# Attention's product with the values, in two runs for each pair of heads instead of one key chunk a slot

## The chip, the core and the metric

One core of one Trainium2 chip (trn2). The time is microseconds of device time for one execution. The core's engines are TensorE (PE in the profile; its weight loads are PEld), VectorE (DVE), ScalarE (ACT), GpSimd (POOL) and SyncE (SP), which issues the DMAs. Each works through its own list of instructions in order; semaphores join them. Matmuls write to PSUM, which has eight banks.

## What is computed

Attention over 4 batches and 8 heads with 576 positions and a head size of 64, followed by two feed-forward layers over the 2304 tokens of width 512. The attention part, cut to what matters here:

```python
scores = scale * np.matmul(q, k.transpose(0, 1, 3, 2)) + bias      # bias: 8 x 576 x 576, one for each head
scores = scores - np.max(scores, axis=-1, keepdims=True)
attn = np.exp(scores)
attn = attn / (np.sum(attn, axis=-1, keepdims=True) + 1e-09)
return np.matmul(attn, v)
```

The first layer is `g = h * cos(h)` between two products, the second an RMS norm with a gated product. Everything is float32.

## The kernel before

The kernel runs in stages: the bias (to about 66 us), attention (about 67 to 366 us), the first layer, the second layer. The change is in the attention stage alone, `attention_phase`.

Attention goes through 16 pairs of heads. The two heads of a pair have 5 query tiles each (four of 128 rows and one of 64), so a pair is 10 tiles and 10 **slots**. In slot s of pair n the engines do this, each in the order written:

- PE: `score` computes tile s into one of two PSUM bank pairs (`scores[s % 2]`), in four matmuls of 288 columns (L505). It first waits until VectorE has finished tile s-2 (semaphore `biased`). Then `turn` transposes the normalised probabilities of the tile of four slots ago (`T_LAG`), with four transposes (L531) and for tiles 5 to 9 a fifth (L527). It waits until the tile is normalised, and until ScalarE has copied the tile two before it out of PSUM (semaphore `copied`), since `turned` has two banks. Then `mix` multiplies one chunk of 128 keys with the values for one half (288) of the queries.
- VectorE: `guard` and `invert` of tile s-2 (L654, L659), `normalise` of tile s-3 where it is an even one (L411; GpSimd has the odd ones), and `add_bias` of tile s (L647), which waits for `scored`.
- ScalarE: `exps` of tile s (L597), which waits for `add_bias` of tile s, then `keep` of tile s-4 (L611, tile 9 also L609), the copy of the transposed tile out of PSUM.
- GpSimd: `normalise` of the odd tiles, and the high and low parts of q and k of what comes next (L346, L350, L356).

Five chunks make one half: chunks 0 to 3 go as two matmuls, one for each head, each of which writes 64 of the 128 PSUM partitions (L550, shape 128*64 in the profile; each shows as two records), and the fifth, with the 64 keys left of both heads, as one matmul over all 128 (L554, shape 128*128). The two halves are 10 chunks for 10 slots: half 0 of pair n-1 in slots 3 to 7, half 1 in slots 8, 9 and 0 to 2 of the next pair. VectorE copies a finished half to `X` (`keep_mixed`, L668) in slots 8 and 3, and the transposed end keys (`keep_end`, L664) after the `add_bias` of slot 4.

After the last pair PE goes through ten slots without scores, then does the first product of the next layer (`chunks.first_h`, L821 to L823), then the last three chunks of half 1. VectorE has `keep_mixed` of the second last pair, `keep_end`, the split of the next layer's input (`features.high`, `features.low`, L808 and L815) and then the last two `keep_mixed`.

Of the kernel before, what the change touches and what calls it, by code (L numbers as in the profile page):

```python
# [29 lines left out]
NQ = 5  # L30
TILES = 2 * NQ
HS = S // 2
QPAD = NQ * P
EXP_LAG, T_LAG = 2, 4
EARLY_TILES = 3


# [21 lines left out]
def after_waits(eng, passed):  # L59


    eng.sem_inc(passed, 1)


def rows_of(qt):

    return P if qt < NQ - 1 else S - (NQ - 1) * P


def bias_phase(nc, sb, sem_of, ins, bias_scratch, att):  # L70
# [43 lines left out]

    EARLY = -(-EARLY_TILES * P // (KINDS * ROWS))
    assert N % 2 == 0 and EARLY % 2 == 0
# [10 lines left out]
    with nc.Block() as block:  # L127

        @block.sync
        def _(sp):  # L130
# [27 lines left out]
            for stored in (*bias_stored[0], *bias_stored[1]):  # L158
                sp.wait_ge(stored, 8 * EARLY)
            for s in range(EARLY_TILES):  # L160
                att.load_bias(sp, 0, s, True, 0)
# [206 lines left out]
def attention_phase(nc, sb, sem_of, att, features, weights, chunks, bank_pairs, banks):  # L368
    ctx = ExitStack()
    X, ident, values, bias = att.X, att.ident, att.values, att.bias  # L370
    scored, biased, mixed_ready = att.scored, att.biased, att.mixed_ready
# [9 lines left out]
    probs_t_end = [sb(ctx, f"probs_t_end{i}", [P, S], F32) for i in range(2)]  # L381
# [8 lines left out]
    copied = sem_of("a_copied")  # L390
    end_copied = sem_of("a_end_copied")
    last_end_copied = sem_of("a_last_end_copied")
    mixed_copied = sem_of("a_mixed_copied")
# [3 lines left out]
    LAST = PAIRS - 1  # L397
# [3 lines left out]
    def normed_of(n, s):  # L401

        return (pool_normed if s in POOL_TILES else dve_normed), n * (TILES // 2) + (s // 2 + 1)
# [10 lines left out]
    with nc.Block() as block:  # L414

        @block.sync
        def _(sp):
            for stored in (*att.bias_stored[0], *att.bias_stored[1]):
                sp.wait_ge(stored, 8 * (GROUPS // KINDS))
            for s in range(EARLY_TILES, TILES):  # L420
                att.load_bias(sp, 0, s, True, 0)
# [73 lines left out]
        @block.tensor  # L495
        def _(pe):
            def score(n, s, first):
                h, qt = s // NQ, s % NQ
                if qt == 0:
                    pe.wait_ge(att.prepared[h], n + 1)  # L500
                if not (first and s < 2):
                    pe.wait_ge(biased, n * TILES + (s - 1))
                for half in range(2):
                    for part, k_part in ((0, att.k_high[h]), (1, att.k_low[h])):
                        last = nc.tensor.matmul(scores[s % 2][:, half, 0:HS], att.q_parts[h][:, qt * P:(qt + 1) * P],  # L505
                                                k_part[:, half * HS:(half + 1) * HS], start=(part == 0), stop=(part == 1))
                last.then_inc(scored, 1)

            def turn(n, s, first):

                h, qt = s // NQ, s % NQ
                rows = rows_of(qt)
                pe.wait_ge(*normed_of(n, s))
                if not (first and s < 2):
                    pe.wait_ge(copied, n * TILES + (s - 1))
                if s == NQ and not first:
                    pe.wait_ge(end_copied, n)
                if h == 1:

                    both = by_heads[qt][0:rows, :, :, :].rearrange("p h a b -> p (h a b)")[:, S - D:S + D]  # L520
                    end = turned[s % 2] if qt == NQ - 1 else turned_end
                    at = (NQ - 1) * rows if qt == NQ - 1 else qt * P
                    pe.wait_ge(*normed_of(n, qt))
                if qt == NQ - 1 and not first:
                    after_waits(pe, pe_passed)
                if h == 1:
                    nc.tensor.transpose(end[:, at:at + rows], both, ident[0:rows, 0:rows])  # L527
                flat = probs[s].rearrange("p a b -> p (a b)")
                for c in range(NQ - 1):
                    at = h * D + c * P  # L530
                    last = nc.tensor.transpose(turned[s % 2][:, c * rows:(c + 1) * rows], flat[0:rows, at:at + P],  # L531
                                               ident[0:rows, 0:rows])
                last.then_inc(turned_ready, 1)

            def mix(n, parity, half, c, first):

                if c == 0:
                    if half == 0:
                        pe.wait_ge(att.values_in[parity], n * 8 + (16 - 8 * parity))

                        pe.wait_ge(copied, n * TILES + (NQ + 3))
                    else:
                        pe.wait_ge(copied, (n + 1) * TILES)
                        pe.wait_ge(last_end_copied, n + 1)
                    if not (first and half == 0):
                        pe.wait_ge(mixed_copied, n * 2 + half)
                queries = slice(half * HS, (half + 1) * HS)
                if c < NQ - 1:
                    for h in range(2):
                        nc.tensor.matmul(mixed[h * D:(h + 1) * D, 0:HS], values[parity][:, c, h, :],  # L550
                                         probs_t[parity][:, h, c, queries], start=(c == 0), stop=False)
                else:
                    pe.wait_ge(end_copied, n + 1)
                    nc.tensor.matmul(mixed[:, 0:HS], values[parity][:, c, :, :].rearrange("p h d -> p (h d)"),  # L554
                                     probs_t_end[parity][:, queries], start=False, stop=True).then_inc(mixed_ready, 1)

            def slot(n, parity, s, step, compute=True):

                if compute:
                    score(n, s, step == 0)  # L560
                if s < T_LAG:
                    if step > 0:
                        turn(n - 1, TILES - T_LAG + s, False)
                elif compute:
                    turn(n, s - T_LAG, step == 0)
                if s < 3:
                    if step > 1:
                        mix(n - 2, parity, 1, s + 2, False)
                elif step > 0:
                    half, c = divmod(s - 3, NQ)  # L570
                    mix(n - 1, 1 - parity, half, c, step == 1)

            def pair(n, parity, step):
                for s in range(TILES):
                    slot(n, parity, s, step)

            pe.wait_ge(att.ident_ready, 2)
            pe.wait_ge(att.pad_ready, 2)
            pair(0, 0, 0)
            pair(1, 1, 1)  # L580
            with pe.Fori(1, PAIRS // 2) as m:
                pair(m * 2, 0, 2)
                pair(m * 2 + 1, 1, 2)
            for s in range(TILES):
                slot(PAIRS, 0, s, 2, compute=False)

            pe.wait_ge(biased, PAIRS * TILES)
            chunks.first_h(pe)
            for c in range(2, NQ):
                mix(LAST, 1, 1, c, False)  # L590

        @block.scalar
        def _(act):
# [44 lines left out]
        def _(dve):  # L638
# [22 lines left out]
            def keep_end(n, parity):  # L661

                dve.wait_ge(turned_ready, n * TILES + (TILES - 1))
                dve.tensor_copy(probs_t_end[parity][:, 0:(NQ - 1) * P], turned_end[:, :]).then_inc(end_copied, 1)  # L664

            def keep_mixed(n, half):
                dve.wait_ge(mixed_ready, n * 2 + (half + 1))
                dve.tensor_copy(X[:, bass.ds(n * S + half * HS, HS)], mixed[:, 0:HS]).then_inc(mixed_copied, 1)  # L668

            def back(n, parity, s, by):  # L670

                return (n, parity, s - by) if s >= by else (n - 1, 1 - parity, TILES + s - by)

            def pair(n, parity, step, hp=None):

                for s in range(TILES):
                    m, _, r = back(n, parity, s, EXP_LAG)
                    m3, _, r3 = back(n, parity, s, EXP_LAG + 1)

                    if step > 1 and s == 3:  # L680
                        keep_mixed(n - 2, 1)
                    if step > 0 and s == 8:
                        keep_mixed(n - 1, 0)
                    if s >= EXP_LAG or step > 0:
                        guard(m, r)
                    if (s >= EXP_LAG + 1 or step > 0) and r3 not in POOL_TILES:
                        normalise(dve, m3, r3, dve_normed)
                    if s >= EXP_LAG or step > 0:
                        invert(m, r)
                    if hp is not None:  # L690
                        dve.wait_ge(att.bias_in[s], (hp + 1) * 16)
                    add_bias(n, s, step == 0)
                    if step > 0 and s == 4:
                        keep_end(n - 1, 1 - parity)

            pair(0, 0, 0, hp=0)
            pair(1, 1, 1)
# [788 lines left out]
```

## Time and profile before

| | |
|---|---|
| median of 3 runs | 1233.66 us (1233.5 to 1233.79) |
| the profiled execution | 1233.59 us |
| its span in the trace | 1231.8 us |
| PE busy | 1192.9 us (97%) |
| PEld busy | 1076.7 us (87%) |
| DVE busy | 701.6 us (57%) |
| ACT busy | 500.5 us (41%) |
| POOL busy | 483.1 us (39%) |

The span is the time from the first to the last instruction in the trace; some 1.8 us lie around it. The busy shares are means over stages of different kinds, so the attention stage has to be read by itself. An engine's busy time is the time in which at least one of its instructions was under way; the ends of matmuls are modelled.

### The profile page before, as it was taken

The numbers are of one execution on the slowest core, as the hardware profiler recorded it, in microseconds if no ns is written. First come the engines' busy times: TensorE is split into PE (matmuls) and PEld (weight loads), VectorE is DVE, ScalarE is ACT, GpSimd is POOL, SyncE is SP. The second block draws the span as 40 slices with busy tenths as digits, with TensorE's granted clock in tenths as the row PEclk, the third lists the DMA queues.
The fourth block names the chain that finished last, engine by engine and source line by source line (L and its number), as shares of the span: only waits on it lengthen the run. The fifth ranks groups of instructions, "written<-read, shape, count | busy, mean of one in ns | idle before, by whom it ended". The sixth has DMA issues, their size and how long they took to land. (4 is left out here: it accounts for less than half of the span.)

```text
span 1231.8 us, 21813 instructions
## 1 busy us (share of the span) xinstructions
PE 1192.9 (97%) x7464; PEld 1076.7 (87%) x7464; DVE 701.6 (57%) x1540; ACT 500.5 (41%) x1034; POOL 483.1 (39%) x515
## 2 busy tenths in 40 slices
PE   5789999999989999999999999999999999999998
PEld 2367777777759999999999999999999999999998
DVE  8977777777759977868686788554002020110201
ACT  6967777777733333334333333211111111111111
POOL 3056666666665452433325254572111111111111
PEclk9989999999989999999999999999999999999999
DMA  5854425252124300000000001241000000000000
GB/s 176 248 167 123 157 79 184 71 166 94 61 67 120 86 2 1 0 0 0 0 0 0 0 17 52 69 137 35 1 1 26 0 26 0 0 26 0 26 0 26
DMA packets 46534, 69.06 MB, mean 56 GB/s; under 512 B 3712, under 2 KB 27424, under 8 KB 46496
## 3 DMA queue, kind: packets, MB, share of 16 engines
q1 hardware_dynamic: 46496, 68.60, 17.9%
q8 instruction: 19, 0.31, 0.1%
q14 instruction: 19, 0.16, 0.0%
HBM read 53.25 MB, written 15.34 MB: 56 GB/s over the span
## 5 line engine op out<-in xcount | busy, mean ns | idle before, releaser
L823 PE MATMUL banks<-x_high,w_low_rest 128*128 128x384 f32 x672 | 224.8, 334 | 0.0
L822 PE MATMUL banks<-x_low,w_high_rest 128*128 128x384 f32 x672 | 224.6, 334 | 0.0
L821 PE MATMUL banks<-x_high,w_high_rest 128*128 128x384 f32 x672 | 224.6, 334 | 0.0
L1370 DVE TENSOR_TENSOR X<-X,banks 128x384 f32<-128x384 f32 x72 | 39.8, 552 | 299.1 <-PE banks L823 299.1
L1389 POOL TENSOR_TENSOR product_low<-X,product_high 128x384 fp32r<-128x384 f32 x72 | 72.8, 1011 | 346.0 <-ACT product_high L1332 346.0
L1187 POOL TENSOR_TENSOR product_low<-g,product_high 128x384 fp32r<-128x384 f32 x96 | 102.4, 1066 | 236.7 <-ACT product_high L1069 236.7
L821 PE MATMUL bank<-product_high,w_high_rest 128*128 128x384 f32 x480 | 162.2, 338 | 0.8 <-POOL product_low L1187 0.8
L823 PE MATMUL bank<-product_high,w_low_rest 128*128 128x384 f32 x480 | 160.7, 335 | 0.0
L822 PE MATMUL bank<-product_low,w_high_rest 128*128 128x384 f32 x480 | 160.6, 335 | 0.0
L647 DVE CUSTOM_DVE_ANT_0 probs<-banks,bias 128x576 f32<-128x576 f32 (+1 forms) x160 | 119.8, 749 | 61.1 <-PE banks L505 59.1
L597 ACT ACTIVATE probs<-probs,neg_max 128x576 f32<-128x576 f32 (+1 forms) x160 | 124.4, 777 | 71.8 <-DVE neg_max L647 71.1
L1097 ACT ACTIVATE angle<-angle,quarter 128x384 f32<-128x384 f32 x96 | 59.3, 617 | 202.6 <-DVE angle L1129 202.6
L823 PEld LDWEIGHTS banks<-x_high,w_low_rest 128*128 128x128 f32 x672 | 126.2, 188 | 0.0
L822 PEld LDWEIGHTS banks<-x_low,w_high_rest 128*128 128x128 f32 x672 | 126.2, 188 | 0.0
L821 PEld LDWEIGHTS banks<-x_high,w_high_rest 128*128 128x128 f32 x672 | 126.2, 188 | 0.0
L505 PE MATMUL banks<-k_high,q_parts 128*128 128x288 f32 x320 | 111.0, 362 | 2.5 <-PEq L127 2.5
L411 POOL TENSOR_SCALAR probs<-probs,inv_total 128x576 f32<-128x576 f32 (+1 forms) x80 | 59.5, 744 | 131.4 <-DVE inv_total L659 130.8
L505 PEld LDWEIGHTS banks<-k_high,q_parts 128*128 128x128 f32 x320 | 61.5, 192 | 56.5 <-DVE neg_max L647 37.5
L1319 ACT ACTIVATE X<-banks 128x384 f32<-128x384 f32 x71 | 34.9, 492 | 185.4 <-PE banks L823 185.4
L1332 ACT ACTIVATE product_high<-X 128x384 fp32r<-128x384 f32 x72 | 37.8, 525 | 172.5 <-DVE X L1370 172.5
L1124 DVE SCALAR_TENSOR_TENSOR angle<-turns,angle 128x384 f32<-128x384 int32 x96 | 105.5, 1099 | 3.1
L550 PE MATMUL bank<-probs_t,values 128*64 128x288 f32 x512 | 90.3, 435 | 4.7 <-DVE X L668 4.7
(113 smaller groups left out, 2547.4 us busy)
## 6 DMA issues: line engine op xcount, KB each, us to landing
raw_qk<-in_qk SPq DMA_DIRECT2D x32, 576.0 KB, 3.7
bias_scratch<-bias_stage SPq DMA_DIRECT2D x36, 288.0 KB, 3.1
bias<-bias_scratch SPq DMA_DIRECT2D x32, 288.0 KB, 3.1
w_raw<-in_w_out SPq DMA_DIRECT2D x28, 256.0 KB, 2.6
values<-in_v SPq DMA_DIRECT2D x16, 320.0 KB, 4.0
w_raw<-in_w_in SPq DMA_DIRECT2D x16, 256.0 KB, 3.0
out_t<-X SPq DMA_DIRECT2D x5, 768.0 KB, 3.5
w_raw<-in_w_gate SPq DMA_DIRECT2D x12, 256.0 KB, 3.0
```

What stands on the lines that cost most here:

```text
L411: eng.tensor_scalar(probs[s][0:rows], probs[s][0:rows], inv_total[0:rows, s:s + 1], scalar2, ALU.mult, op1).then_inc(normed, 1)
L505: last = nc.tensor.matmul(scores[s % 2][:, half, 0:HS], att.q_parts[h][:, qt * P:(qt + 1) * P], k_part[:, half * HS:(half + 1) * HS], star ...
L550: nc.tensor.matmul(mixed[h * D:(h + 1) * D, 0:HS], values[parity][:, c, h, :], probs_t[parity][:, h, c, queries], start=(c == 0), stop=False)
L597: act.activation(probs[s][0:rows], probs[s][0:rows], ACT.Exp, bias=neg_max[0:rows, s:s + 1], scale=-1.0, accum_out=total[0:rows, s:s + 1]) ...
L647: dve.tensor_tensor_reduce(out=probs[s][0:rows], in0=scores[s % 2][0:rows, :, 0:HS], in1=bias[s][0:rows, :, :], scale=-float(D) ** -0.5, s ...
L821: nc.tensor.matmul(out, high, x_high, start=start, stop=False)
L822: nc.tensor.matmul(out, high, x_low, start=False, stop=False)
L823: return nc.tensor.matmul(out, low, x_high, start=False, stop=stop)
L1097: act.activation(angle[:, :], angle[:, :], ACT.Sin, bias=quarter[:, :]).then_inc(cos_ready, 1)
L1124: dve.scalar_tensor_tensor(angle[:, :], turns[:, :], -TWO_PI_LOW, angle[:, :], ALU.mult, ALU.add).then_inc(fine_angle, 1)
L1187: pool.tensor_tensor(gl[f % 2][:, :], g[:, :], gh[f % 2][:, :].bitcast(F32), ALU.subtract).then_inc(g_split, 1)
L1389: pool.tensor_tensor(sl[f % 2][:, :], s, sh[f % 2][:, :].bitcast(F32), ALU.subtract).then_inc(s_split, 1)
```

## The change

`mix` now issues all five chunks of a half in one go. Half 0 of pair n-1 runs in slot 4 of pair n and half 1 in slot 9, each after the slot's `score` and `turn`. The other eight slots have no product with the values. VectorE's `keep_mixed` moves from slots 3 and 8 to slots 1 and 6, and `keep_end` from behind the `add_bias` of slot 4 to the head of slot 3. After the last pair PE has five slots without scores instead of ten, then `first_h`, then the whole of the last half.

```diff
+MIX_SLOTS = (4, 9)
@@ tensor engine
-            def mix(n, parity, half, c, first):
-
-                if c == 0:
-                    if half == 0:
-                        pe.wait_ge(att.values_in[parity], n * 8 + (16 - 8 * parity))
-
-                        pe.wait_ge(copied, n * TILES + (NQ + 3))
-                    else:
-                        pe.wait_ge(copied, (n + 1) * TILES)
-                        pe.wait_ge(last_end_copied, n + 1)
-                    if not (first and half == 0):
-                        pe.wait_ge(mixed_copied, n * 2 + half)
+            def mix(n, parity, half, first):
+
+                pe.wait_ge(att.values_in[parity], n * 8 + (16 - 8 * parity))
+                pe.wait_ge(copied, n * TILES + (NQ + 3) if half == 0 else (n + 1) * TILES)
+                if not (first and half == 0):
+                    pe.wait_ge(mixed_copied, n * 2 + half)
                 queries = slice(half * HS, (half + 1) * HS)
-                if c < NQ - 1:
+                for c in range(NQ - 1):
                     for h in range(2):
                         nc.tensor.matmul(mixed[h * D:(h + 1) * D, 0:HS], values[parity][:, c, h, :],
                                          probs_t[parity][:, h, c, queries], start=(c == 0), stop=False)
-                else:
-                    pe.wait_ge(end_copied, n + 1)
-                    nc.tensor.matmul(mixed[:, 0:HS], values[parity][:, c, :, :].rearrange("p h d -> p (h d)"),
-                                     probs_t_end[parity][:, queries], start=False, stop=True).then_inc(mixed_ready, 1)
+                pe.wait_ge(end_copied, n + 1)
+                if half == 1:
+                    pe.wait_ge(last_end_copied, n + 1)
+                nc.tensor.matmul(mixed[:, 0:HS], values[parity][:, NQ - 1, :, :].rearrange("p h d -> p (h d)"),
+                                 probs_t_end[parity][:, queries], start=False, stop=True).then_inc(mixed_ready, 1)
@@ slot
-                if s < 3:
-                    if step > 1:
-                        mix(n - 2, parity, 1, s + 2, False)
-                elif step > 0:
-                    half, c = divmod(s - 3, NQ)
-                    mix(n - 1, 1 - parity, half, c, step == 1)
+                if step > 0 and s in MIX_SLOTS:
+                    mix(n - 1, 1 - parity, MIX_SLOTS.index(s), step == 1)
@@
-            for s in range(TILES):
+            for s in range(MIX_SLOTS[0] + 1):
                 slot(PAIRS, 0, s, 2, compute=False)
 
             pe.wait_ge(biased, PAIRS * TILES)
             chunks.first_h(pe)
-            for c in range(2, NQ):
-                mix(LAST, 1, 1, c, False)
+            mix(LAST, 1, 1, False)
@@ vector engine
-                    if step > 1 and s == 3:
+                    if step > 1 and s == 1:
                         keep_mixed(n - 2, 1)
-                    if step > 0 and s == 8:
+                    if step > 0 and s == 6:
                         keep_mixed(n - 1, 0)
+                    if step > 0 and s == T_LAG - 1:
+                        keep_end(n - 1, 1 - parity)
...
                     add_bias(n, s, step == 0)
-                    if step > 0 and s == 4:
-                        keep_end(n - 1, 1 - parity)
```

## Rows read from the trace of the kernel before

**Rows 1.** Stretches: busy us and instructions of each engine, PE clock, DMA share, GB/s

```profile
74.00:86.00 12.00, 10.00 (x74) 8.49 (x72) 11.73 (x40) 10.88 (x27) 9.73 (x11) 1.00 0.36 122
193.00:210.70 17.70, 17.70 (x123) 12.53 (x121) 13.46 (x50) 13.13 (x32) 11.95 (x13) 1.00 0.65 204
357.00:364.00 7.00, 6.50 (x22) 4.75 (x24) 0.35 (x1) 0.00 (x0) 1.72 (x2) 0.51 0.29 77
```

**Rows 2.** PE timeline, first score matmul of slot 0, two pairs: start us, us, what

```profile
97.69 0.40 PE L505 MATMUL banks<-k_high,q_parts 128*128 128x288 f32 x1
115.38 0.40 PE L505 MATMUL banks<-k_high,q_parts 128*128 128x288 f32 x1
```

**Rows 3.** PE timeline: a slot with a two-head chunk, one with the end chunk

```profile
211.59 0.29 PE L505 MATMUL banks<-k_low,q_parts 128*128 128x288 f32 x1
211.72 0.60 PE L531 MATMUL bank<-ident,probs 128*128 128x128 f32 x4
212.25 0.71 PE L550 MATMUL bank<-probs_t,values 128*64 128x288 f32 x4
212.89 0.40 PE L505 MATMUL banks<-k_high,q_parts 128*128 128x288 f32 x1
...
217.57 0.65 PE L554 MATMUL bank<-probs_t_end,values 128*128 128x288 f32 x2
...
218.19 0.29 PE L505 MATMUL banks<-k_low,q_parts 128*128 128x288 f32 x1
```

**Rows 4.** PE timeline behind the last pair: four two-head chunks back to back

```profile
350.09 2.16 PE L550 MATMUL bank<-probs_t,values 128*64 128x288 f32 x16 [0.18 <-DVE X L668]
...
352.18 0.75 PE L554 MATMUL bank<-probs_t_end,values 128*128 128x288 f32 x2
```

**Rows 5.** Timeline of pairs 0 and 1, slots without any product with the values

```profile
74.62 0.78 ACT L597 ACTIVATE probs<-probs,neg_max 64x576 f32<-64x576 f32 x1 [0.18 <-DVE neg_max L647]
...
75.40 0.57 ACT L611 ACTIVATE probs_t<-bank 128x512 f32<-128x512 f32 x1
...
76.12 0.63 PE L531 MATMUL bank<-ident,probs 128*128 128x128 f32 x4 [0.44 <-ACT probs_t L611]
...
84.47 0.78 ACT L597 ACTIVATE probs<-probs,neg_max 128x576 f32<-128x576 f32 x1
...
85.73 0.76 ACT L597 ACTIVATE probs<-probs,neg_max 128x576 f32<-128x576 f32 x1
```

**Rows 6.** Timeline of VectorE and the exp behind it, steady pairs and pair 15

```profile
212.10 0.75 DVE L647 CUSTOM_DVE_ANT_0 probs<-banks,bias 64x576 f32<-64x576 f32 x1 [0.45 <-PE banks L505]
...
212.79 0.07 DVE L647 DVE_READ_ACCUMULATOR2_ANT neg_max<- 64x1 f32 x1
...
212.90 0.78 ACT L597 ACTIVATE probs<-probs,neg_max 64x576 f32<-64x576 f32 x1 [0.22 <-DVE neg_max L647]
...
213.39 0.14 DVE L654 TENSOR_SCALAR guarded<-total 128x1 f32<-128x1 f32 x1
...
213.95 0.73 DVE L647 CUSTOM_DVE_ANT_0 probs<-banks,bias 128x576 f32<-128x576 f32 x1
...
342.29 0.46 DVE L668 COPY X<-bank 128x288 f32 x1
...
343.12 0.76 DVE L647 CUSTOM_DVE_ANT_0 probs<-banks,bias 128x576 f32<-128x576 f32 x1
```

**Rows 7.** Timeline of the end of the stage

```profile
345.53 0.33 PE L527 MATMUL bank<-ident,probs 128*128 128x128 f32 x1
...
349.86 0.68 DVE L664 COPY probs_t_end<-bank 128x512 f32<-128x512 f32 x1
...
357.50 0.75 PE L550 MATMUL bank<-probs_t,values 128*64 128x288 f32 x2 [4.56 <-DVE X L668]
...
366.42 0.19 PEld L821 LDWEIGHTS banks<-x_high,w_high_head 128*128 128x128 f32 x1 [1.25 <-issue]
```

**Rows 8.** VectorE's normalise in the view of line L411: duration ns min/median/max

```profile
L411 DVE TENSOR_SCALAR probs<-probs,inv_total x80: 501/510/1233, 72.3 to 346.4; 128x576 f32<-128x576 f32 x64, 64x576 f32<-64x576 f32 x16
```

## The prediction

> **What bounds the kernel now.** The page gives PE 97% of the span, but the change touches one stage only, so I read the stretches by stage first, then the timeline of single slots, then the few places where the trace already shows what the changed kernel will do everywhere. In a steady pair PE is busy for all of its 17.70 us, while DVE has 13.46, ACT 13.13 and POOL 11.95 [rows 1]. Pair follows pair every 17.69 us (97.69 to 115.38) [rows 2]. So today PE sets the pace and waits for nobody; every slot is about 1.8 us long, and each of the others idles a little in each slot. Note for later that PE's weight loads cover only 12.53 of 17.70.
>
> Where does PE's time go? In a slot with a two-head chunk the transposes start at 211.72, the chunk at 212.25 (0.53 later) and the next scores at 212.89 (0.64 later) [rows 3]. In a run of four such chunks, which the tail of the stage has, they take 350.09 to 352.18, 2.09 us, or 0.52 each [rows 4]. Each single chunk pays at its two borders as well: the end chunk, which has the shape of its neighbours, goes from its start at 217.57 to the second score matmul at 218.19, 0.62 for two records and one score matmul of 0.13 (211.59 to 211.72), so 0.49 of streaming [rows 3].
>
> **The change part by part.**
>
> *PE's own work.* A slot with a two-head chunk is 0.36 longer than one with the end chunk counted at its streaming time: 0.10 ahead of it (0.53 where four transposes at 0.11 need 0.43), 0.15 in it (0.64 less 0.49) and 0.11 in the slower first score behind it [rows 3]. Eight such slots a pair pay 2.9 us. In the new form a run pays once: 0.10 ahead, 2.09 for the four chunks instead of 1.96, and 0.10 in the end chunk (its two records take 0.75 behind a run and 0.65 else [rows 3, 4]), some 0.4 a half and 0.8 a pair. PE's own work falls by 2.1 us, to 15.6 a pair. This part is sure; the same instructions ran in the same order in the tail.
>
> *What the others must do in the meantime.* Now the slots differ: eight have 0.96 to 1.07 us of PE work, two have about 3.7. DVE and ACT cannot store work for the long slots: `scores` has two buffers, so when PE goes into a run they have at most the tile just scored and the one before it. And in the short slots they are slower than PE. Pair 0 and the first slots of pair 1 show exactly such slots, without any product: in 74 to 86 us DVE is busy 11.73 of 12, ACT 10.88, PE 10.00 [rows 1]. There PE waits for ACT's copy: the exp of a slot starts at 74.62, the copy behind it at 75.40, and the turn of two slots later can start at 76.12 [rows 5]. So **exp of slot s to turn of slot s+2 is 1.50**, and a backlogged ACT starts an exp every 1.26 (84.47 to 85.73) [rows 5].
>
> From these I walk once round the loop. Half A, from the turn of slot 4 to the turn of slot 9:
> - turn of slot 4 to the run: 0.53. The run: 2.09. End chunk to the last score matmul of slot 5: 0.62 + 2 x 0.13 + 0.10 behind a run = 0.98. Last score matmul to `add_bias` on an idle DVE: 0.51 (211.59 to 212.10). Sum 4.11 [rows 3, 4, 6].
> - `add_bias` to exp of slot 5: 0.80 (212.10 to 212.90) [rows 6].
> - slot 5 to slot 6, with `keep_mixed` now at the head of slot 6: 0.69 to the end of `add_bias` (212.10 to 212.79) and 0.83 from the copy to the next `add_bias` (342.29 to 343.12), 1.52, and the exp follows at the same distance [rows 6].
> - slot 6 to 7: ACT's 1.26. Exp of slot 7 to turn of slot 9: 1.50 [rows 5].
> - Half A: 4.11 + 0.80 + 1.52 + 1.26 + 1.50 = 9.19.
>
> Half B, from the turn of slot 9 to that of the next slot 4: a fifth transpose (0.11) makes the first term 4.22; then 0.80; slot 0 to 1 has both `keep_mixed` and an even tile to normalise, 0.69 + 0.46 + 0.56 (guard at 213.39 to `add_bias` at 213.95) = 1.71 [rows 6]; then 1.26 and 1.50. Half B: 9.49.
>
> **One pair: 18.68 us, 0.99 longer than now** (17.69), although PE has 2.1 less to do. PE would be idle for 3.1 of it. I take 18.65.
>
> *Other waits.* `keep_end` stands in DVE's slot 3 now, 0.68 ahead of that slot's `add_bias`; that `add_bias` is not on the loop (slot 2's exp is), and PE needs the copy only 2.09 into the run. The run of half 1 needs the last copy of slot 3, five slots before. `keep_mixed` never waits, because a run is through before the next slot's scores. POOL has 11.95 in 18.65; its normalise of tile 5, needed by the turn of slot 9, comes after slot 7's `invert`, and a POOL instruction takes 0.92 in the mean (11.95 for 13 [rows 1]), against 2.3 us until that turn (0.80 and 1.50). The loads of q, k, values and bias wait for the same steps as now, with a longer pair. All these at nothing; if one more POOL step lands ahead of it, the price is another 0.92 at most, in a pair where that happens.
>
> *The page on packing.* ACT's copies get PSUM free at a rate of 10 x 1.26 = 12.6 us a pair, below PE's new 15.6 [rows 5]. The Trainium skill, TensorEngine Tiling (Array Packing), PSUM Bottleneck, says that tiling quickens TensorE but not the evacuation, which may become the limit. Taken as a rate it would not bind here and the pair would be 15.6; what I expect is its delay, not its rate.
>
> *Start.* In pair 1 the exp of slot 2 starts at 85.73 in both kernels, so the turn of slot 4 comes at 87.23 [rows 5]. Fourteen pairs on it is 87.23 + 14 x 18.65 = 348.33; the turn of slot 9 of the last pair 9.19 later, 357.52; behind its run (0.64 + 2.09 + 0.59) the turn of tile 6, 360.84. Now that turn is at 345.53 [rows 7]. **15.3 us lost by then.**
>
> *Tail.* Now the stage needs 20.9 us from that turn to the next stage's first load at 366.42. Within it VectorE starts `keep_end` 4.33 in (349.86), finishes the split of the input at about 357.0 (`keep_mixed`'s 0.46 [rows 6] ahead of PE's start at 357.50), 11.5 in, and PE waits 4.56 for that `keep_mixed`, because half 1's first chunks stand ahead of `first_h`; then it works at half the clock, 0.51 granted [rows 1, 7]. In the new order no chunk stands there. Slots without chunks let `keep_end` start about 2.3 in (estimate: two turns, with 1.5 from turn over copy to turn, by the durations of [rows 5]), the split ends 7.1 later, as now (349.86 to 357.0), at 9.4; `first_h` follows it piece by piece and ends at 10.1; the run 2.1, end chunk, `keep_mixed` and the exit together 1.7: about 13.9. **7.0 us won.** If the clock falls to 1.2 GHz as it does now (half of 2.4), `first_h`'s end and the run take twice as long and the gain is 4.2. I take 7.0, because PE no longer stands still for 4.56 but does a quarter of `first_h` for each of the four parts that VectorE has split (L815), and the clock kept 1.00 with 2 of 12 us idle in pair 0 [rows 1].
>
> Sum against the profiled execution: 1233.59 + 15.3 - 7.0 = 1241.9. The median of the runs is 0.07 above that execution, so 1242.0.
>
> **The rivals.**
>
> *PE stays the bound (faster).* If DVE and ACT keep up, because PE's waits in pair 0 are few (0.44 is the one in [rows 5]) and the loop is shorter than I add up, a pair takes 15.6. Then fourteen pairs save 14 x 2.1 = 29.4, pair 1 about 1, the tail 7: 1196. For it: PE is the one engine without idle time. Against: the loop's terms are all measured, and would have to be 3 us a pair too long. It decides where half a loop falls under 7.8. The Trainium skill, Perfetto Trace Analysis, Identifying the Most-Contended Engine, gives this result: improve the engine of highest occupancy first, though it wants TensorE judged by its weight loads, whose share here is 12.53 of 17.70 [rows 1].
>
> *The bubbles are smaller.* If the loop is 0.5 to 1 us shorter, because in places a `keep_mixed` or the exp of slot 6 is hidden behind the wait for the scores, the pair is as long as now and the tail's gain is left over: 1227 to 1235.
>
> *The loop is longer.* VectorE's normalise takes 0.51 by the median, but up to 1.23 [rows 8], which I put down to GpSimd working beside it, and in the new order the normalise of slots 1 and 7 is on the loop. By my order POOL is idle or waiting at both, but if one of them is hit, each pair gains 0.6 more, 14 x 0.6 = 8: 1250. The half clock in the tail alone gives 1245.
>
> **How the numbers follow.** Loop as walked: 0.70, own range 1236 to 1248 (0.35 a pair either way and the clock). PE the bound or nearly: 0.09. Smaller bubbles: 0.11. Longer loop: 0.10. 0.2% is 2.5 us, about what a measurement of this kernel can tell from no change. Faster by more than that: 0.09 and half of the smaller bubbles, 0.14. Within it: 0.07. Slower: 0.79. The range takes in the main case and most of both neighbours: 1231 to 1251.
>
> **What would show it.** Right: a steady pair of about 18.65 us with PE busy some 15.6; PE idle ahead of the turns of slots 4 and 9, released by ACT's copy (L611), in all some 3 us a pair; DVE idle for about 1.5 to 2.5 us ahead of the `add_bias` of slots 5 and 0, released by the scores; runs of 2.09 for L550; the turn of tile 6 behind the last pair near 360.8 and the next stage 13 to 17 us after it. Wrong: a pair below 17.7, or idle time that stands elsewhere (POOL's normalise, DMA), or L550 records longer than 0.26 apart in a run.

## The result and the profile after

The changed kernel takes 1239.71 us, median of 4 runs (1239.44 to 1240.08); the kernel before, on the same chip, 1233.58. The ratio is 1.0056, with a 95% interval of 1.0044 to 1.0068: slower by 0.56%, or some 6.9 us by the ratio (6.1 by the two medians). The profiled execution took 1239.96 us, its span 1238.2, so 6.4 us more than the span before.

The head of the page of the changed kernel, busy time of each engine:

```profile
span 1238.2 us, 21829 instructions
PE 1176.5 (95%) x7464; PEld 1079.6 (87%) x7464; DVE 698.5 (56%) x1540; ACT 494.1 (40%) x1034; POOL 482.6 (39%) x515
```

The same number of instructions on each of these engines, 16.4 us less of PE, and a longer time: PE did save work and now stands still elsewhere. The same view as [rows 1], one steady pair (18.52 us) and the tail:

```profile
193.00:211.52 18.52, 16.84 (x123) 12.88 (x122) 13.23 (x48) 12.75 (x31) 11.93 (x14) 1.00 0.66 197
363.00:370.00 7.00, 5.91 (x34) 3.26 (x32) 5.72 (x6) 2.09 (x4) 6.75 (x7) 1.00 0.41 112
```

PE was busy for all of 17.70 us and now is for 16.84 of 18.52. Who waits for whom in the pairs between 140 and 317 us (total in us, times, longest):

```profile
POOL probs L412 <- DVE inv_total L650: 60.4, 48, 2.7
ACT probs L588 <- DVE neg_max L638: 53.5, 48, 2.4
DVE probs L638 <- PE banks L506: 43.8, 19, 2.7
...
PE bank L532 <- ACT probs_t L602: 5.9, 10, 0.6
PE bank L528 <- ACT probs_t L602: 3.9, 10, 0.5
```

The third row shows it best. VectorE waits for scores only 19 times, twice a pair, but for 2.3 us each: once behind every run. Before, it waited a little in many slots, 0.45 in the one shown in [rows 6]. The last two rows are new, PE waiting for ScalarE's copies; before, that was to be seen only in pairs 0 and 1 [rows 5].

Now one half of the loop, from the turn of slot 4 (198.82) to the turn of slot 9 (207.96), in the timeline of the changed kernel. L532 and L528 are the transposes, L545 the two-head chunks, L550 the end chunk, L638 `add_bias`, L588 exp:

```profile
198.82 0.63 PE L532 MATMUL bank<-ident,probs 128*128 128x128 f32 x4
...
199.38 2.16 PE L545 MATMUL bank<-probs_t,values 128*64 128x288 f32 x16
...
201.47 0.75 PE L550 MATMUL bank<-probs_t_end,values 128*128 128x288 f32 x2
...
202.97 0.76 DVE L638 CUSTOM_DVE_ANT_0 probs<-banks,bias 128x576 f32<-128x576 f32 x1 [1.99 <-PE banks L506]
...
203.77 0.78 ACT L588 ACTIVATE probs<-probs,neg_max 128x576 f32<-128x576 f32 x1 [2.23 <-DVE neg_max L638]
...
204.38 0.29 PE L506 MATMUL banks<-k_low,q_parts 128*128 128x288 f32 x1
...
204.47 0.76 DVE L638 CUSTOM_DVE_ANT_0 probs<-banks,bias 128x576 f32<-128x576 f32 x1
...
205.27 0.63 PE L532 MATMUL bank<-ident,probs 128*128 128x128 f32 x4 [0.60 <-ACT probs_t L602]
205.27 0.78 ACT L588 ACTIVATE probs<-probs,neg_max 128x576 f32<-128x576 f32 x1
...
206.52 0.76 ACT L588 ACTIVATE probs<-probs,neg_max 128x576 f32<-128x576 f32 x1
...
207.96 0.30 PE L528 MATMUL bank<-ident,probs 128*128 128x128 f32 x1
```

Read it downwards: turn to run 0.56, the run 2.09, end chunk to `add_bias` 1.50, to the exp 0.80, to the next exp 1.50 (the copy of a finished half stands between the two `add_bias`), to the next 1.25, and from there to the turn 1.44. Sum 9.14. While VectorE (1.99) and ScalarE (2.23) wait, PE is in its run; then PE waits for them.

The tail, which answers to [rows 7]:

```profile
359.57 0.27 PE L528 MATMUL bank<-ident,probs 128*128 128x128 f32 x1
...
361.79 0.69 DVE L655 COPY probs_t_end<-bank 128x512 f32<-128x512 f32 x1 [1.56 <-PE bank L532]
...
363.40 4.95 DVE L806 TENSOR_TENSOR x_low<-X,x_high 128x384 fp32r<-128x384 f32 x4
...
365.18 0.41 PE L812 MATMUL banks<-x_high,w_high_head 128*128 128x384 f32 x1 [0.20 <-DVE x_low L806]
...
369.12 2.16 PE L545 MATMUL bank<-probs_t,values 128*64 128x288 f32 x16
...
372.78 0.41 PE L812 MATMUL banks<-x_high,w_high_head 128*128 128x384 f32 x1 [0.82 <-PEq L415]
```

The turn of tile 6 behind the last pair is at 359.57, 14.0 us later than before (345.53). From there the next stage starts after 13.2 us instead of 20.9. 14.0 - 7.7 = 6.3, and the spans differ by 6.4.

### The profile page after: what moved, and what is told of

Same layout as the page of the kernel before. It is cut to its first block and busy times, and to the rows that moved or that the text cites. A ratio compares the mean times of both kernels' runs of the same rounds, so it can differ in the third digit from the quotient of the medians.

```text
span 1238.2 us, 21829 instructions
## 1 busy us (share of the span) xinstructions
PE 1176.5 (95%) x7464; PEld 1079.6 (87%) x7464; DVE 698.5 (56%) x1540; ACT 494.1 (40%) x1034; POOL 482.6 (39%) x515
## 5 line engine op out<-in xcount | busy, mean ns | idle before, releaser
L638 DVE CUSTOM_DVE_ANT_0 probs<-banks,bias 128x576 f32<-128x576 f32 (+1 forms) x160 | 119.4, 747 | 78.0 <-PE banks L506 71.3
L588 ACT ACTIVATE probs<-probs,neg_max 128x576 f32<-128x576 f32 (+1 forms) x160 | 123.6, 773 | 90.7 <-DVE neg_max L638 88.4
L506 PE MATMUL banks<-k_high,q_parts 128*128 128x288 f32 x320 | 107.9, 352 | 3.0 <-PEq L128 2.5
L532 PE MATMUL bank<-ident,probs 128*128 128x128 f32 (+1 forms) x640 | 91.1, 264 | 14.9 <-ACT probs_t L602 9.5
L812 PEld LDWEIGHTS bank<-product_high,w_high_rest 128*128 128x128 f32 x480 | 90.1, 188 | 2.1 <-POOL product_low L1178 1.1
```

Source lines behind the costliest of these rows:

```text
L588: act.activation(probs[s][0:rows], probs[s][0:rows], ACT.Exp, bias=neg_max[0:rows, s:s + 1], scale=-1.0, accum_out=total[0:rows, s:s + 1]) ...
L638: dve.tensor_tensor_reduce(out=probs[s][0:rows], in0=scores[s % 2][0:rows, :, 0:HS], in1=bias[s][0:rows, :, :], scale=-float(D) ** -0.5, s ...
L812: nc.tensor.matmul(out, high, x_high, start=start, stop=False)
```

## The experiments

The length of a pair is taken in each trace as the distance of the `add_bias` of slot 5 in successive pairs, mean over pairs 3 to 15. Times are medians; each ratio is to the kernel before, run on the same chip (1232.39 us beside the first four experiments, 1232.93 beside the last four), with its 95% interval.

| kernel | time, us | ratio | pair, us |
|---|---|---|---|
| before | 1233.58 | 1 | 17.70 |
| changed | 1239.71 | 1.0056 (1.0044 to 1.0068) | 18.53 |
| before, new tail | 1228.01 | 0.9964 (0.995 to 0.9979) | 17.70 |
| changed, `keep_mixed` in slots 3 and 8 | 1231.06 | 0.9989 (0.9979 to 0.9998) | 17.94 |
| changed, copy ahead of exp | 1222.80 | 0.9927 (0.9911 to 0.9944) | 17.25 |
| before, copy ahead of exp | 1232.78 | 1.0002 (0.9993 to 1.0012) | 17.70 |
| four runs a pair | 1224.43 | 0.9934 (0.9918 to 0.9951) | 17.48 |
| four runs, copy ahead of exp | 1209.62 | 0.9811 (0.9795 to 0.9827) | 16.47 |
| changed, runs of half the length | 1212.72 | 0.9835 (0.9819 to 0.9852) | 16.60 |
| changed, copy ahead of exp, `keep_end` behind slot 3 | 1220.55 | 0.9897 (0.9881 to 0.9914) | 17.09 |

The theory was that a loop of waits sets the pair, and that the tail is a gain of its own. The rival was that some engine's amount of work does.

**The tail alone.**

```diff
--- before
-            for s in range(TILES):
+            for s in range(8):
                 slot(PAIRS, 0, s, 2, compute=False)
             pe.wait_ge(biased, PAIRS * TILES)
             chunks.first_h(pe)
-            for c in range(2, NQ):
+            for c in range(NQ):
                 mix(LAST, 1, 1, c, False)
```

> The kernel before, with the new tail alone: one key chunk a slot in all pairs, and behind the last pair the slots end with half 0, then comes first_h, then the whole of half 1. Theory (the tail is a gain of its own, which hides part of what the runs cost): PE no longer waits 4.56 us for keep_mixed ahead of first_h, first_h follows the split of the input, the last half runs at full clock; the stage ends about 5 us earlier (366.4 to about 361.6), so about 1229. Rival (the tail's gain needs the runs, or the split of the input on VectorE alone sets the stage's end): no more than 1 us, 1232.5 to 1233.7.

Measured: 1228.01, 4.4 us less. Its timeline has the last half at 357.82 and GpSimd, which starts the next stage with the others (366.41 in the kernel before), at 361.44:

```profile
357.82 2.16 PE L550 MATMUL bank<-probs_t,values 128*64 128x288 f32 x16
...
359.91 0.75 PE L554 MATMUL bank<-probs_t_end,values 128*128 128x288 f32 x2
...
361.44 0.10 POOL L1206 MEMSET quarter<- 128x1 f32 x1 [2.57 <-POOLq L414]
```

The last half ran in 2.09 (357.82 to 359.91), as the run behind the last pair in [rows 4] did, and the granted clock from 357 to 361.4 is 1.00. So this gain of the tail does not need the runs; it hid part of their price in the result. It is 5.0 us on the timeline (366.41 to 361.44), of the 7.7 that the changed kernel wins there. The other 2.7 I put down to the slots that have no chunk: there `keep_end` starts 2.2 us behind the turn of tile 6 instead of 4.3.

**`keep_mixed` off the loop.**

```diff
--- changed kernel
-                    if step > 1 and s == 1:
+                    if step > 1 and s == 3:
                         keep_mixed(n - 2, 1)
-                    if step > 0 and s == 6:
+                    if step > 0 and s == 8:
                         keep_mixed(n - 1, 0)
```

> The changed kernel with keep_mixed back in VectorE's slots 3 and 8 instead of 1 and 6; the runs stay. Theory (a loop of waits from the turn of one run's slot over add_bias, exp and copy to the turn of the next run's slot sets the pair): keep_mixed stands on that loop in slots 1 and 6. Without it slot 5 to 6 costs ScalarE's 1.26 instead of 1.52 and slot 0 to 1 costs 1.26 instead of 1.71, so the pair falls by 0.7, from 18.52 to about 17.8, and the time by 14 to 15 times that, to about 1229. Rival (PE's or VectorE's amount of work sets the pair): the same copies are made, no change, 1239 to 1240.

Measured: 1231.06, and 17.94 a pair, 0.59 less than the changed kernel. The same copies, made two slots later, are worth 8 us (the ratios differ by 0.0067). An engine's amount of work cannot explain that; their place on the loop can. The walk had 0.7 and 1229.

**ScalarE's copy ahead of its exp**, in the changed kernel and in the one before.

```diff
--- changed kernel, and kernel before
                 for s in range(TILES):
-                    exps(n, s)
                     if s >= T_LAG:
                         keep(n, parity, s - T_LAG)
                     elif not first:
                         keep(n - 1, 1 - parity, TILES - T_LAG + s)
+                    exps(n, s)
```

> The changed kernel, with ScalarE's two steps of each slot in the other order: the copy of tile s-4 out of PSUM first, then the exp of tile s. Nothing is added or left out. Theory (the loop of waits): the copy that frees the bank for the turn two slots later no longer stands behind the exp of the tile just scored. By the same walk half A falls to about 8.3 and half B to about 8.2, the pair from 18.5 to about 16.5, the time to about 1210 (1206 to 1218). Rival (ScalarE's or VectorE's amount of work, or the wait for the scores, sets the pair): ScalarE has the same work, no change within 2 us of 1239.7.

> The kernel before with the same swap of ScalarE's copy and exp. Theory: with one chunk a slot PE is the bound and waits for nobody, so the order on ScalarE is worth nothing in the steady pairs; only pair 0 and the first slots of pair 1, where PE waits for the copies, get up to 3 us shorter: 1230.5 to 1233.8. Rival (the order on ScalarE is worth something by itself): 1225 or less, or slower because each exp now starts later.

Measured: 1222.80 and 17.25 a pair in the changed kernel, so 1.28 us a pair for an order alone; 1232.78 and the same 17.70 in the kernel before. The swap is worth nothing where PE is the bound and 16 us where the loop is (1.0056 less 0.9927). But the walk had promised 2.0 a pair, and 1222.80 is outside its range of 1206 to 1218. The trace of the swapped kernel shows what came up in its place, at the turn of slot 4:

```profile
189.92 0.69 DVE L655 COPY probs_t_end<-bank 128x512 f32<-128x512 f32 x1
...
190.52 0.14 DVE L645 TENSOR_SCALAR guarded<-total 128x1 f32<-128x1 f32 x1
190.58 0.51 DVE L412 TENSOR_SCALAR probs<-probs,inv_total 128x576 f32<-128x576 f32 x1
...
191.15 0.66 PE L532 MATMUL bank<-ident,probs 128*128 128x128 f32 x4 [0.25 <-DVE probs L412]
```

The turn waits for VectorE's normalise, and that stands behind `keep_end`, which the change had moved to the head of slot 3. So I moved it behind the slot's `add_bias`:

```diff
--- changed kernel with the copy ahead of the exp
-                    if step > 0 and s == T_LAG - 1:
-                        keep_end(n - 1, 1 - parity)
...
                     add_bias(n, s, step == 0)
+                    if step > 0 and s == T_LAG - 1:
+                        keep_end(n - 1, 1 - parity)
```

> The changed kernel with ScalarE's copy ahead of the exp (1222.8, 17.23 a pair instead of the 16.5 of my walk), and keep_end moved behind the add_bias of slot 3. In the trace of that kernel the turn of slot 4 waits for VectorE's normalise of tile 0, which stands behind keep_end (0.69) in slot 3. Theory (with the copy off the loop, VectorE's slot 3 is what the turn of slot 4 waits for): the wait of 0.25 to 0.3 goes and the pair falls to about 16.95, the time to about 1218.5. Rival (the scores that wait for VectorE's add_bias set that turn anyway): no change, 1222 to 1223.5.

Measured: 1220.55, 17.09 a pair: 0.16 of the 0.3 expected. The placement costs something, but the rest up to the walk's 16.5 is not there. No run takes the remaining 0.6 apart. The trace shows one wait that the walk did not have: in both swapped kernels PE stops for 0.87 us a pair ahead of score matmuls, until VectorE's `add_bias` of two tiles before has freed the banks; in the changed kernel it is 0.25 (by the starts, as counted under the next heading).

**Runs of half the length.**

```diff
--- changed kernel
-                for c in range(NQ - 1):
+                for c in range(2):
                     for h in range(2):
                         nc.tensor.matmul(mixed[h * D:(h + 1) * D, 0:HS], ...
```

> The changed kernel without chunks 2 and 3 of both halves: each run is two two-head chunks and the end chunk. What is left out: the product with 256 of the 576 keys, so the time is read as that of a shorter run only. Theory (a run lies on the loop of waits in full): two chunks are 0.97 us by the spacing of 0.243 for two records, so a pair is 1.94 shorter, 16.6 against 18.52, and the time 1209 to 1212. Rival (ScalarE or VectorE is the bound by its amount of work, and hides a part of the run): the pair stays above 17.5, 1224 or more.

Measured: 16.60 a pair, 1.93 less than 18.53 where 1.94 was expected, and 1212.72 in all. The time is a little above the expected 1209 to 1212. A microsecond taken from a run is a microsecond off the pair, down to 16.6; ScalarE's or VectorE's amount of work, which is the same here, is not the bound at 18.5. PE's own work would give the same fall; that it is not the bound either is shown by the two swaps of place and order above, which leave PE's work as it is, and by the 3.0 us a pair for which PE stops in this kernel as well, by the starts. The view by stretches shows VectorE and ScalarE below 13.3 in 16.60:

```profile
193.00:209.60 16.60, 14.80 (x106) 11.66 (x106) 13.19 (x49) 12.73 (x32) 11.96 (x13) 1.00 0.56 191
```

**Four runs a pair instead of two.** Two chunks in slot 3 and the rest of half 0 in slot 5; the same for half 1 in slots 8 and 0. `mix` now takes the chunks that it is to do; its own lines are left out below.

```diff
--- changed kernel
+            PARTS = {3: (0, (0, 1)), 5: (0, (2, 3, 4)), 8: (1, (0, 1)), 0: (1, (2, 3, 4))}
...
-                if step > 0 and s in MIX_SLOTS:
-                    mix(n - 1, 1 - parity, MIX_SLOTS.index(s), step == 1)
+                if s in PARTS:
+                    half, part = PARTS[s]
+                    if s == 0:
+                        if step > 1:
+                            mix(n - 2, parity, half, False, part)
+                    elif step > 0:
+                        mix(n - 1, 1 - parity, half, step == 1, part)
...
-            for s in range(MIX_SLOTS[0] + 1):
+            for s in range(6):
                 slot(PAIRS, 0, s, 2, compute=False)
...
-                    if step > 1 and s == 1:
+                    if step > 1 and s == 2:
                         keep_mixed(n - 2, 1)
-                    if step > 0 and s == 6:
+                    if step > 0 and s == 7:
                         keep_mixed(n - 1, 0)
```

> The changed kernel with each half's run cut in two: chunks 0 and 1 of half 0 in slot 3, chunks 2, 3 and the end chunk in slot 5; of half 1 in slot 8 and in slot 0 of the next pair. keep_mixed goes to VectorE's slots 7 and 2. Theory (a short run is covered by the two score buffers): behind a run of two chunks PE's own work up to the turn three slots on (5.8 us) is longer than the loop of waits (5.0), behind one of two chunks and the end chunk it is 4.6 against 5.4. In sum 17.2 us a pair, where PE's own work is 16.3, so below the 17.7 of the kernel before, and with the tail's 5 us some 1221 (1217 to 1226). Rival (any bunching costs, because the others cannot follow): 18 or more a pair, 1232 or more.

> The same four runs a pair, with ScalarE's copy ahead of its exp in each slot. Theory: the wait for the copy is what is left above PE's own work of 16.3, and goes: 16.4 to 16.8 a pair, so 1209 to 1216. Rival (what is left is VectorE's or the scores' part of the loop): as the four runs alone, within 3 us.

Measured: 1224.43 and 17.48 a pair, above the 17.2 and inside the range of the time; with the copy ahead of the exp 1209.62 and 16.47 a pair. The last is the fastest of all, 1.9% below the kernel before. One of its pairs:

```profile
193.00:209.47 16.47, 16.43 (x123) 12.74 (x121) 13.43 (x51) 13.30 (x32) 12.14 (x14) 1.00 0.49 167
```

PE is busy for 16.43 of 16.47 again: the loop is gone and PE's own work is the bound, and that is where the price of the borders shows. Four runs instead of eight single chunks save four borders at 0.36, 1.44, and 17.70 - 1.44 = 16.26. The measured 16.47 is 0.2 above it; PE still stops for 0.3 a pair by the starts (0.2 in the kernel before).

## Why the prediction was right

It gave 1242.0, in 1231 to 1251, with 0.79 on slower; the result is 1239.71, and in its own main range. By its steps:

- *PE's own work falls by 2.1 a pair.* The busy time of PE does not show it, since the ends of matmuls are modelled and each stop hides a part of itself behind one. The starts do. I count as a stop what the distance of two starts has beyond 0.13 from a score matmul to the turn, beyond 0.03 from a turn to the next scores, and beyond the usual distance inside a turn; these are the distances where nothing holds PE. The turn of slot 7, at 205.27 above, comes 0.89 behind the score matmul at 204.38: a stop of 0.76, shown as 0.60. The next two turns:

```profile
206.13 0.29 PE L506 MATMUL banks<-k_low,q_parts 128*128 128x288 f32 x1
...
206.72 0.43 PE L532 MATMUL bank<-ident,probs 64*128 64x64 f32 x4 [0.29 <-issue]
...
207.58 0.29 PE L506 MATMUL banks<-k_low,q_parts 128*128 128x288 f32 x1
```

  That is 0.46 (206.13 to 206.72, less 0.13) and 0.25 (207.58 to 207.96, less 0.13). From pair 3 to pair 15 the stops are 3.0 us a pair, and 0.2 in the kernel before, so PE's own work is 15.5 against 17.5: 2.0 less. In the fastest kernel it is 16.2, so four borders saved are 1.36, or 0.34 each, where the prediction had 0.36. The run in a pair takes the 2.09 of the tail, to the digit.
- *The loop.* Half A was 9.19, measured 9.14, with no term off by more than 0.06. Half B was 9.49; 18.53 less 9.14 leaves 9.39. The one term I had put too high is slot 0 to slot 1: I charged the whole 0.46 of `keep_mixed`, but the next instruction starts before it ends. Next, slots 0 and 1 of the changed kernel, 193.70 to 195.31, 1.61 instead of 1.71:

```profile
193.70 0.76 DVE L638 CUSTOM_DVE_ANT_0 probs<-banks,bias 128x576 f32<-128x576 f32 x1 [2.65 <-PE banks L506]
...
194.39 0.45 DVE L659 COPY X<-bank 128x288 f32 x1
...
194.75 0.13 DVE L645 TENSOR_SCALAR guarded<-total 64x1 f32<-64x1 f32 x1
...
195.31 0.73 DVE L638 CUSTOM_DVE_ANT_0 probs<-banks,bias 128x576 f32<-128x576 f32 x1
```

- *`keep_end` at nothing.* So in the steady pairs. In pair 1 the turn of slot 4 came at 87.65 instead of 87.23, and waited for the normalise behind `keep_end`. But that normalise took 1.65 us there, where its median is 0.51; with 0.51 it would have ended at 86.46, before ScalarE's copy at 86.88, which that turn needs too. So it took both, the place of `keep_end` and one slow normalise; why that one was slow no run shows.

```profile
85.29 0.69 DVE L655 COPY probs_t_end<-bank 128x512 f32<-128x512 f32 x1
...
85.95 1.65 DVE L412 TENSOR_SCALAR probs<-probs,inv_total 128x576 f32<-128x576 f32 x1
...
86.30 0.58 ACT L602 ACTIVATE probs_t<-bank 128x512 f32<-128x512 f32 x1
...
87.65 0.66 PE L532 MATMUL bank<-ident,probs 128*128 128x128 f32 x4 [0.50 <-DVE probs L412]
```

- *The sum to the end of the pairs.* 15.3 predicted, 14.0 measured. Fourteen rounds at 18.53 instead of 18.65 are 1.7 less; the late first turn gives 0.4 back.
- *The tail.* 7.0 predicted, 7.7 measured. The choice I had to make was the clock, and it went as taken: 1.00 granted from 363 to 370, where the kernel before had 0.51 in 357 to 364. `keep_end` starts 2.2 us behind the turn, where I had estimated 2.3. A quarter of `first_h` follows each part of the split, with waits of 0.2 and more, and the clock held through them. This is 2.4 GHz against 1.2 before; what differs ahead of it is 4.56 us of nothing before, and pieces of work here, as in the kernel before with the new tail, which kept 1.00 too.
- *The rivals.* PE as the bound would have been 1196. The longer loop did not come: the normalises of slots 1 and 7 took 0.50 or 0.51 in every pair from 2 to 15; longer ones (0.76 to 0.84 in slot 5 and 0.98 to 1.08 in slot 9, in pairs 2 to 14) stand off the loop. The Trainium skill's advice to improve the engine of highest occupancy first (Perfetto Trace Analysis, Identifying the Most-Contended Engine) points at PE, correctly as the kernel before stands: its work is what set the pair. That the next bound is a delay no occupancy shows: in the changed kernel the occupancies of PE, VectorE and ScalarE in a pair are 0.91, 0.71 and 0.69. The Trainium skill's remark that PSUM evacuation may become the limit (TensorEngine Tiling (Array Packing), PSUM Bottleneck) names the place of the new wait. As a rate evacuation is not the limit of the changed kernel: ScalarE does the same copies in 16.47 us a pair in the fastest one.
- *The signs.* PE was to be busy for 15.6 a pair and idle for 3.1. By the starts it is 15.5 and 3.0; the busy time of the view has 16.84 and 1.68, so it was the wrong place to look. Time that PE loses in short stops has to be taken from starts. What I had wrong without harm is where the stops stand: ahead of the turns of slots 4 and 9 there is only 0.4 of them. Most of the rest is ahead of slots 7 and 8 (1.2) and 2 and 3 (1.0). The wait for the copy is the one I had named, exp of slot s to turn of slot s+2 (203.77 to 205.27 is 1.50), but PE meets it first behind the exp of slot 5, ahead of slot 7's turn, and stops there already. VectorE's waits ahead of the `add_bias` of slots 5 and 0, put at 1.5 to 2.5, are 1.99 and 2.65.

## What to carry to other kernels

Work that is spread thin over the slots of a loop in which the engines wait for each other also lets the other engines follow. Before it is bunched, walk once round from the end of a bunch over all engines to the start of the next, in starts of a trace; if that is longer than the saved round, shorten the bunch, and take off the walk what need not be on it (here four short runs and the copy ahead of the exp: 0.9811 of the kernel before, against 1.0056 with two long runs as written). And look at the part behind the loop on its own: the tail here was a gain of 4.4 us that needed none of it.

## What the runs showed that I had not expected

The swap of ScalarE's two steps was worth 0 us with PE as the bound, 1.28 a pair with two runs and 1.01 a pair with four (17.48 to 16.47). The 1.01 is more than the four runs gain without it (17.70 to 17.48). It had been the step that I took for fixed.
